# A fused recurrent-attention and expert kernel: two products of each pair of heads as one full matmul instead of two tiled ones

## The reference, cut to what matters

```python
for t in range(S):
    y[:, :, t] = np.einsum('bhd,bhde->bhe', rt, state)
    Sa = np.einsum('bhde,bhe->bhd', state, at)
    state_decay = state * wt[:, :, None, :] - np.einsum('bhd,bhe->bhde', Sa, bt)
    state = state_decay + np.einsum('bhd,bhe->bhde', vt, kt)
...
x = y as (tokens, 320)
h = (x @ w1) * (x @ w2) @ w3;  x = h @ w_out          # 320 -> 1024 -> 1024 -> 320
h = np.maximum(x @ w_in, 0.0); out = h * h @ w_out2   # 320 -> 2048 -> 320
```

## Time and profile before

| | |
|---|---|
| median of 3 runs | 1100.99 us (1100.59 to 1103.22) |
| the profiled execution | 1100.62 us, span 1098.1 us |
| PE busy | 1052.2 us, 96% |
| PE weight loads | 895.0 us, 81% |
| DVE / POOL / ACT busy | 634.2 / 553.1 / 415.1 us |
| mean granted PE clock | 0.984 |

### The profile page before, as it was taken

The page is one execution under the profiler, slowest core; times in us unless marked ns, Lnnn a source line. Parts: engine busy times, 40 slices in busy tenths (PEclk is TensorE's granted clock), DMA queues, the critical chain, the costliest instruction groups (busy, mean ns, idle before and its releaser), DMA issues.

```text
span 1098.1 us, 27872 instructions
## 1 busy us (share of the span) xinstructions
PE 1052.2 (96%) x11056; PEld 895.0 (81%) x11056; DVE 634.2 (58%) x987; ACT 415.1 (38%) x771; POOL 553.1 (50%) x1573
## 2 busy tenths in 40 slices
PE   6989689999989999999999999999999999999998
PEld 5767678778868888888888888888888888898897
DVE  7848256677757556656546657556566556333333
ACT  3444234344434234334234334224334234332232
POOL 4778727537555364585374575473675463600000
PEclk9999699999999999999999999999999999999999
DMA  9944367666768646647645658645557543546552
GB/s 169 190 101 92 84 182 201 157 170 188 190 201 229 148 135 150 151 147 196 158 138 136 151 154 204 156 130 141 148 160 202 146 136 103 156 144 227 180 166 76
DMA packets 269504, 172.74 MB, mean 157 GB/s; under 512 B 201792, under 2 KB 231488, under 8 KB 269376
## 3 DMA queue, kind: packets, MB, share of 16 engines
q1 hardware_dynamic: 269376, 170.97, 59.9%
HBM read 144.18 MB, written 26.74 MB: 156 GB/s over the span
## 4 chain that ended last, share of the span: by engine, by line
PE 77%; DVE 3%; issue 2%; SPq 2%; ACT 1%; DMA 0%; DVEq 0%; ACTq 0%
PE aside L854 30%; PE moe_bank L922 15%; PE moe_bank L907 9%; PE both L816 3%; PE both L717 3%; PE both L758 2%; PE both L750 2%; PE both L831 2%; PE both L827 2%; PE both L799 2%; PE both L701 1%; PE both L730 1%; PE both L840 1%; PE both L781 1%; PE both L807 1%
## 5 line engine op out<-in xcount | busy, mean ns | idle before, releaser
L656 POOL TENSOR_TENSOR inv_tmp<-blk,inv 128x60 f32<-128x60 f32 (+24 forms) x744 | 244.4, 328 | 252.2 <-DVE blk L1428 195.2
L660 POOL TENSOR_TENSOR inv<-inv,inv_tmp 128x60 f32<-128x60 f32 (+24 forms) x744 | 265.6, 357 | 58.3
L922 PE MATMUL moe_bank<-v_ring,h_hi 128*128 128x320 f32 x768 | 178.7, 320 | 0.0
L1508 DVE TENSOR_TENSOR hidden<-left 128x512 f32<-128x512 f32 x96 | 67.9, 707 | 129.6 <-ACT left L1216 129.6
L854 PE MATMUL aside<-xT_hi,w_ring 128*128 128x512 f32 x480 | 132.8, 406 | 0.1
L854 PE MATMUL aside<-x2T_hi,w_ring 128*128 128x512 f32 x480 | 132.7, 406 | 0.0
L922 PEld LDWEIGHTS moe_bank<-v_ring,h_hi 128*128 128x128 f32 x768 | 128.2, 190 | 3.3
L1496 DVE TENSOR_TENSOR h_lo<-hidden,h_hi 128x512 fp32r<-128x512 f32 x144 | 99.0, 688 | 48.1 <-ACT h_hi L1204 47.5
L1216 ACT ACTIVATE left<-aside 128x512 f32<-128x512 f32 x96 | 57.3, 597 | 172.2 <-PE aside L854 102.6
L922 PE MATMUL moe_bank<-v_ring,h_lo 128*128 128x320 f32 x384 | 119.2, 310 | 0.0
L1204 ACT CAST h_hi<-hidden 128x512 fp32r<-128x512 f32 x144 | 89.5, 621 | 77.0 <-DVE hidden L1504 38.4
(11 more groups left out here) (146 smaller groups left out, 1605.3 us busy)
## 6 DMA issues: line engine op xcount, KB each, us to landing
w_ring<-gate_rows SPq DMA_DIRECT2D x40, 640.0 KB, 4.6
w_ring<-win_rows SPq DMA_DIRECT2D x40, 640.0 KB, 4.1
v_ring<-wout_rows SPq DMA_DIRECT2D x80, 320.0 KB, 3.0
v_ring<-fold_rows SPq DMA_DIRECT2D x48, 384.0 KB, 4.1
gate_rows<-w_ring SPq DMA_DIRECT2D x8, 640.0 KB, 3.8
win_rows<-w_ring SPq DMA_DIRECT2D x8, 640.0 KB, 4.1
wout_rows<-v_ring SPq DMA_DIRECT2D x16, 320.0 KB, 2.8
stage<-in_moe_w SPq DMA_DIRECT2D x8, 512.0 KB, 4.9
```

The lines of the kernel that those rows point to most:

```text
L656: nc.gpsimd.tensor_tensor(tmp, x[:, j, 0:j].unsqueeze(2).broadcast_to([P, j, X - lo]), mine[:, j:j + 1, lo:X].broadcast_to([P, j, X - lo]) ...
L660: nc.gpsimd.tensor_tensor(mine[:, 0:j, lo:X], mine[:, 0:j, lo:X], tmp, ALU.add).then_inc(solve, 1)
L922: last = nc.tensor.matmul(bank(f"o{s}")[:, 0:M], h[at % RING][:, s * P:(s + 1) * P], weights[:, rest * M:(rest + 1) * M], start=f == 0 and ...
L1508: nc.vector.tensor_tensor(hidden[x % 2][:], left[x % 2][:], left[x % 2][:], ALU.mult).then_inc(squared, 1)
```

## The change

make_z multiplies both heads of a pair at once: per pair one matmul with all 128 columns of azk as weights and the 80 columns of both heads of zv moving. The result is 128 x 80; of it the two diagonal blocks (first head's rows with the first 40 columns, second head's rows with the last 40) are read. Pair x writes at column 128 x, so both banks are used.

make_y does the same twice per pair: 104 columns of weights, 128 columns moving, once for the state part, once for the chunk part. So that the weights are one contiguous piece, `bk_row` becomes 104 columns a pair (with 24 zero columns between the heads, cleared once at the start), and `st` holds the second head's rows 64 columns further right than the first's.

The readers take the blocks apart: copy_x, copy_rows, copy_state (ACT) and scale_y (DVE) become two instructions each, one per head. Since make_y now also writes the second bank, turn_state waits for `y_scaled` of its own window, and in the opening it is called one step later; turn_w waits for `x_copied` there instead of `rows_copied`.

```diff
@@ -31,7 +31,7 @@
         self.sT = [sb(f"sT{h}", [P, X, D]) for h in range(2)]
-        self.st = [sb(f"st{h}", [P, X, D]) for h in range(2)]
+        self.st = [sb(f"st{h}", [P, X * D + DP]) for h in range(2)]
         self.zeros = sb("zeros", [P, 1])
@@ -126,7 +126,7 @@
         bkT = [sb(f"bkT{h}", [P, X, 2, C]) for h in range(2)]
-        bk_row = [sb(f"bk_row{h}", [P, X, 2, D]) for h in range(2)]
+        bk_row = [sb(f"bk_row{h}", [P, X, E]) for h in range(2)]
         n10 = [sb(f"n10{x}", [P, X, BLK]) for x in range(4)]
@@ -675,7 +675,7 @@
                 if n <= OPENING:
-                    wait(pe, rows_copied, n - 1)
+                    wait(pe, x_copied, n - 1)
                 elif n == OPENING + 1:
@@ -745,10 +745,9 @@
                 for x in range(X):
-                    for q in range(2):
-                        rows = slice(0, P if q == 0 else E)
-                        last = nc.tensor.matmul(its_first(n)[half_rows(q), x * D:(x + 1) * D], azk[half][rows, x, q, :],
-                                                zv[half][rows, x, q, :], start=True, stop=True)
+                    last = nc.tensor.matmul(its_both(n)[:, x * P:x * P + 2 * D],
+                                            azk[half][:, x].rearrange("e q t -> e (q t)"),
+                                            zv[half][:, x].rearrange("e q d -> e (q d)"), start=True, stop=True)
                 last.then_inc(z_made, 1)
@@ -804,7 +803,7 @@
                     for q in range(2):
-                        last = nc.tensor.matmul(its_first(n)[half_rows(q, D), x * D:(x + 1) * D], bk_row[half][:, x, q, :],
+                        last = nc.tensor.matmul(its_first(n)[half_rows(q, D), x * D:(x + 1) * D], bk_row[half][:, x, half_rows(q, D)],
                                                 uv[half][:, x, q, 0:D], start=True, stop=True)
@@ -822,18 +821,20 @@
                 for x in range(X):
-                    for q in range(2):
-                        rows = half_rows(q, D)
-                        nc.tensor.matmul(its_first(n)[rows, x * C:(x + 1) * C], st[half][rows, x, :], rbd_of(n)[rows, x, q, :],
-                                         start=x == 0, stop=False, skip_group_check=True)
+                    nc.tensor.matmul(its_both(n)[0:E, x * P:(x + 1) * P],
+                                     st[half][0:E, x * D:x * D + E],
+                                     rbd_of(n)[0:E, x].rearrange("e q t -> e (q t)"),
+                                     start=x % (X // 2) == 0, stop=False, skip_group_check=True)
                 for x in range(X):
-                    for q in range(2):
-                        last = nc.tensor.matmul(its_first(n)[half_rows(q, D), x * C:(x + 1) * C], bk_row[half][:, x, q, :],
-                                                ruv[:, x, q, :], start=False, stop=True, skip_group_check=True)
+                    last = nc.tensor.matmul(its_both(n)[0:E, x * P:(x + 1) * P],
+                                            bk_row[half][:, x],
+                                            ruv[:, x].rearrange("s q t -> s (q t)"),
+                                            start=False, stop=True, skip_group_check=True)
                 last.then_inc(y_made, 1)
...
                 pe.wait_ge(state_new, n + 1)
+                pe.wait_ge(y_scaled, n + 1)
                 for x in range(X):
@@ -1015,8 +1016,8 @@
             make_y(0)
+            make_x1(1)
             turn_state(0)
-            make_x1(1)
             turn_rows(2)
@@ -1031,8 +1032,8 @@
             make_y(1)
+            cross(4)
             turn_state(1)
-            cross(4)
             turn_rows(3)
@@ -1050,8 +1051,8 @@
             make_y(2)
+            make_u1(3)
             turn_state(2)
-            make_u1(3)
             turn_rows(4)
@@ -1060,8 +1061,8 @@
             make_y(3)
+            multiply_w3(6, 2)
             turn_state(3)
-            multiply_w3(6, 2)
             turn_ar(5)
@@ -1138,11 +1139,15 @@
                 act.wait_ge(turned_rows, n + 1)
-                nc.scalar.copy(bk_row[n % 2][:], by_pair(n)[:, :, :, 0:D]).then_inc(rows_copied, 1)
+                nc.scalar.copy(bk_row[n % 2][:, :, half_rows(0, D)], by_pair(n)[:, :, 0, 0:D])
+                nc.scalar.copy(bk_row[n % 2][:, :, half_rows(1, D)], by_pair(n)[:, :, 1, 0:D]).then_inc(rows_copied, 1)
 
...
                 act.wait_ge(z_made, n + 1)
-                nc.scalar.copy(x_row[n % 2][:], by_head(its_first(n), slice(0, P))).then_inc(x_copied, 1)
+                for q in range(2):
+                    made = its_both(n)[half_rows(q)].rearrange("s (x c) -> s x c", x=X)
+                    last = nc.scalar.copy(x_row[n % 2][half_rows(q)], made[:, :, D * q:D * (q + 1)])
+                last.then_inc(x_copied, 1)
 
@@ -1171,7 +1176,10 @@
                 act.wait_ge(turned_state, n + 1)
-                nc.scalar.copy(st[n % 2][0:E], by_head(its_second(n), slice(0, E))).then_inc(st_copied, 1)
+                for q in range(2):
+                    rows = half_rows(q, D)
+                    last = nc.scalar.copy(st[n % 2][rows, DP * q:DP * q + X * D], its_second(n)[rows, 0:X * D])
+                last.then_inc(st_copied, 1)
 
@@ -1467,8 +1475,11 @@
                 wait(dve, y_stored[n % 2], 64 * (n // 2))
-                nc.vector.tensor_tensor(y_out[n % 2][0:E], by_head(its_first(n), slice(0, E), C), decay[n % 4][0:E, :, 0:C],
-                                        ALU.mult).then_inc(y_scaled, 1)
+                for q in range(2):
+                    rows = half_rows(q, D)
+                    last = nc.vector.tensor_tensor(y_out[n % 2][rows], by_pair(n, rows)[:, :, q, :],
+                                                   decay[n % 4][rows, :, 0:C], ALU.mult)
+                last.then_inc(y_scaled, 1)
 
@@ -1561,12 +1572,14 @@
             nc.vector.memset(zeros[:], 0.0).then_inc(padded, 1)
+            for t in bk_row:
+                nc.vector.memset(t[:, :, D:DP], 0.0).then_inc(padded, 1)
             for x in range(4):
...
                                 unit_rows.rearrange("i y r x -> i y (r x)")).then_inc(unit_turned, 1)
-            dve.wait_ge(padded, 10)
+            dve.wait_ge(padded, 12)
             scan(0)
...
             scale_a(0)
```

## The result

The changed kernel takes 1142.66 us (median of 5 runs, 1139.39 to 1146.73); the kernel before took 1100.99 (5 runs, 1098.34 to 1103.22). The ratio is 1.039, with a 95% interval of 1.0359 to 1.0421: slower by 41.7 us, where 24.6 were forecast and the range ended at 1134. The profiled execution took 1144.71 us, its span is 1143.0, 44.9 more than before.

The account below looks back on a forecast made before the run. PE, busy 96% of the span, was taken to bound the kernel. make_y +26.0, make_z -1.9, opening +1.5 and absorbed -1.0 gave +24.6 on 1100.62; with 0.4 for the median, 1125.6 us, range 1117 to 1134.

Parts of the forecast that it names:

- What bounds the kernel: From 330 to 990 us PE waits for nobody, so added PE work goes into the time at full price.
- make_y: On PE, 2.19 us a window before and 3.49 after: +1.30 a window, 26.0 us over 20 windows.
- make_z: On PE, 1.21 us before and 1.11 after, at 0.072 us a step: -0.10 a window, -1.9 us over 19.
- the 0.15 us that the forecast gave them: Cost on PE of changing the tiling at a tiled group's edges, 0.09 + 0.06 us, expected to vanish with full matmuls.
- The upper end (0.089): Step in us of L730, with 128 weight columns and 104 moving; at it make_z would cost +0.17 us a window.
- The other engines: Doubled scale_y on DVE and doubled copies on ACT stay covered behind PE work: cost 0.
- The opening: Windows 0 to 3: PE's idle until 118.21 us absorbs some 4 us; work added after it counts, +1.5 us.
- the middle case of the clock: In the opening, PE's clock comes back during y(2): stated as +1.3 us, held likeliest and taken as +1.5.
- Around 304 us: PE's 5.2 us wait for a decay behind late loads absorbs added work: -1.0 us, kept open from 0 to -3.6.
- The one on weight loads: Rival: loads bound make_z; at L730's step 5 us more, 1131, chance 10%; at the skill's 107 ns 1137, 2%.

Follow-up runs that it names:

- the four-tile run: The kernel before with make_z in four column tiles of 32 instead of two of 64: 1096.17 us, ratio 0.996.
- the other order in the opening: The changed kernel with turn_uv(3) ahead of turn_rows(4) and multiply_w3(6, 3) ahead of turn_ar(5): 1140.65 us, ratio 1.0364.

## Why the prediction was wrong

**What bounds the kernel**: right. PE works nearly all of 330 to 990 us in both kernels, and each product's added time on PE went into the windows in full: make_y's groups and edges grew by 1.22 us and make_z's group by 0.72, together 1.94, which is what a window grew by.

**make_y**: right. The step of 0.109 us was forecast as 0.111, the group 3.41 instead of 3.49, the difference +1.25 instead of +1.30.

**make_z**: this is the step that failed. The forecast took the step by the moving columns alone, 0.072 us between L685 and L730, and -0.10 us a window. Measured: 0.113 us and +0.69. The group itself grew by 0.72, from 1.06 to 1.78 us, and the edges stayed as they were on the mean. So of the 0.79 us between the two, 0.67 are the step (1.78 against the 1.11 forecast) and the rest are edges: the 0.15 us that the forecast gave them was read at make_y and doesn't hold at make_z. Over 19 windows that is 19 x 0.79 = 15.0 us of the 20.3 that the forecast of the span missed (17 in the medians). The upper end (0.089) was taken from a transpose, which isn't the same form; the nearest plain rows with 128 weight columns, make_read and cross, have 128 columns moving as well and hide the load. The rows of before did hold the answer: pairs of make_z's tiles step at 0.058 us with only 40 columns moving, where make_y's pairs with 64 moving step at 0.056. A pair with fewer moving columns was the slower one, and only its weights were wider. I computed both numbers and didn't ask why.

The Trainium skill (TensorE: Matmul & The Clock Gate, LDWEIGHTS) puts a load at its columns over 1.2 per ns, by which I estimate 107 ns for 128 columns and 87 for 104. The plain f32 matmuls agree with it within 7 ns (0.111 to 0.113 us for 128 columns, 0.089 to 0.093 for 104); the transposes do not (0.089 for 128). The forecast gave this rule a chance of 2% because of L730, and the row held against it was another form.

**The other engines**: right in the loop. Both doubled readers and turn_state's wait cost 0.02 us a window.

**The opening**: mis-sized, +1.5 forecast. Its own terms give +0.9 for the middle case of the clock (5.9 - 2.1 - 2.9), not the +1.3 that it states. That case came true: the clock was at one half from 119.3 to 129.5 us instead of to 134.4, and rose within make_y(2). Window 3's y came 4.8 us later. By rows, y(2) cost +1.9 (1.4 forecast), y(3) +1.5 (1.3) and z(4) +0.75 (-0.1), the last by the same step as the other make_z. PE waited 0.88 us before turn_state and 1.03 behind it, of which the forecast had 0.5: the step behind turn_state needs its copy, and no step lies between them any more. PE's work also began 0.95 us later (119.16 against 118.21), which need not be the change's doing: in the four-tile run, whose make_y is the old one, y(2) starts 0.76 us later than before too.

Window 4 took 2.9 us beyond its 1.9, with the waits of 0.50 and 1.29 us in it, and with 3.4 us at half clock from 167.1 on, which cost 1.7. Both kernels have PE's wait of 2.3 us ahead of that place, and only the changed one the stretch. That it is due to the change isn't shown: the kernel with turn_rows as plain matmuls, which has none of the change, has one at 162.6 us, and the one with 72 weight columns has none.

**Around 304 us**: 2.0 absorbed, 1.0 forecast; window 7 takes 49.30 us as before (49.32). This term moves by itself: with the other order in the opening window 7 took 51.65 us, with a wait of 4.6 us and twice the time at half clock behind it.

**Sum**: 24.6 forecast, + 15.0 for z, - 1.0 for y, + 6.2 for the opening with window 4, - 1.0 for what was absorbed, + 0.5 at the end: 44.3 of the 44.9 us between the two profiled spans.

**Rivals**: none of them was this. The one on weight loads had the mechanism, and priced it at the transpose's step (+0.17) or, by the skill, at +0.50; measured is +0.69. The range took its end from the first. One reading of the forecast was too wide, without effect on the sum: two instructions for each f32 matmul hold for attention alone. The experts' operands are cast to fp32r, and their matmuls stand as one each (L854: 5 + 3 for 8).

## What to carry to other kernels

Joining two small matmuls into one large one with unread blocks pays only if the array had idle room. Here two tiles side by side left none, and each plain f32 step cost the larger of its weight columns and its moving columns. Before pricing a new shape, fit both sides on rows of the same form (a transpose is another), and where two rows of before disagree with a one-sided price, as make_z's tiles did, follow that up first. A matmul bound by its weights can gain from narrower column tiles, as make_z did (1.06 to 0.73 us), since tiles side by side load at once.

## What the runs showed of the hardware

- Plain f32, full width: 128 weight columns step at 0.111 to 0.113 us with 40, 80 and 128 columns moving; 104 at 0.093 with 80 and 0.089 to 0.091 with 64; 72 at 0.064 with 64 and 0.071 with 80, where the moving side takes over.
- Column tiles load in parallel: 64 weight columns in each of two tiles step at 0.058 us a pair, 32 in each of four at (0.80 - 0.21)/63 x 4 = 0.037 us a round, which is what 40 moving columns need (0.036). Instructions to different tiles start 0.009 us apart on the mean.
- A transpose with 128 weight columns and 104 moving steps at 0.089 us, a plain matmul of the same operands at 0.109 and with twice the instructions: 1.05 us more a group (1.70 against 0.65).
